# Router logits taken from the product that turns attention outputs back, in a chained attention, expert and feed-forward kernel

## The reference, cut to what matters

```python
y = attention(q, k, v, a_re, a_im)          # 4 batches, 8 heads, 768 positions, 48 columns
x = y.transpose(0, 2, 1, 3).reshape(3072, 384)
do_compute = (x @ w_skip) > 0               # rows that go to an expert
logits = x @ w_gate                         # 8 experts
e_idx = argmax(logits, axis=1)
gate = softmax(logits)[e_idx]
x[do_compute] += gate * (relu(x @ w1[e_idx]) @ w2[e_idx])
h = x @ w_in
out = (h * sigmoid(h)) @ w_out              # 384 -> 2048 -> 384
```

## Time and profile before

| | |
|---|---|
| median of 3 runs | 878.77 us (878.76 to 878.89) |
| the profiled execution | 878.05 us, of which 876.3 us in the span |
| TensorE busy, whole span | 830.9 us (95%) |
| VectorE, ScalarE, GpSimd busy | 357.0, 347.1, 160.6 us |
| mean granted TensorE clock | 0.985 of full speed |
| attention and routing, about | 0 to 298 us |
| experts' first product | from 306.65 us |

### The profile page before, as it was taken

One profiled execution on the slowest core, in us unless ns is written; L12 is line 12 of the kernel. 1 busy time (PEld: TensorE's weight loads), 2 busy tenths in 40 slices (PEclk: granted clock), 3 DMA queues, 4 the chain that ended last, 5 costly groups with the idle time before them and its releaser, 6 DMA issues.

```text
span 876.3 us, 13204 instructions
## 1 busy us (share of the span) xinstructions
PE 830.9 (95%) x5194; PEld 744.6 (85%) x5194; DVE 357.0 (41%) x668; ACT 347.1 (40%) x606; POOL 160.6 (18%) x193
## 2 busy tenths in 40 slices
PE   1499999999999799999999999999999999999997
PEld 0277887798899589999998989998999889988997
DVE  1598878868765422223413122132122122122112
ACT  6889988888652131111112222222222222222221
POOL 2101122712503305555300001001001001001001
PEclk9699999999999899999999999999999999999999
DMA  9999778666523496899720001000000000000001
GB/s 171 160 205 244 105 99 123 113 94 83 136 94 117 140 202 167 266 233 252 224 73 1 1 0 37 1 1 37 1 1 36 1 1 37 1 1 37 0 1 37
DMA packets 174165, 77.31 MB, mean 88 GB/s; under 512 B 151592, under 2 KB 167304, under 8 KB 174096
## 3 DMA queue, kind: packets, MB, share of 16 engines
q1 hardware_dynamic: 169168, 60.54, 34.4%
q0 software_dynamic: 4928, 15.84, 6.4%
HBM read 60.80 MB, written 15.59 MB: 87 GB/s over the span
## 4 chain that ended last, share of the span: by engine, by line
PE 91%; DVE 3%; issue 2%; ACT 2%; DMA 1%; POOL 0%; SPq 0%; DVEq 0%; ACTq 0%; POOLq 0%
PE f_pU L1698 23%; PE f_pO L1704 22%; PE e_pH L1434 9%; PE e_pY L1448 8%; PE sc L515 5%; PE kvp L529 3%; PE tq L497 2%; PE tk L502 2%; PE yp L540 2%; PE yp L542 2%; PE cs L472 2%; PE cs L110 2%; PE cs L485 1%; PE cs L486 1%; PE cs L92 1%
## 5 line engine op out<-in xcount | busy, mean ns | idle before, releaser
L1698 PE MATMUL f_pU<-f_xT,wi 128*128 128x512 f32 x864 | 215.1, 395 | 0.8 <-DVE f_xT L1639 0.8
L1704 PE MATMUL f_pO<-wo,gT 128*128 128x384 f32 x1152 | 213.8, 336 | 0.0
L1704 PEld LDWEIGHTS f_pO<-wo,gT 128*128 128x128 f32 x1152 | 202.6, 188 | 7.5
L1698 PEld LDWEIGHTS f_pU<-f_xT,wi 128*128 128x128 f32 x864 | 161.3, 188 | 32.5 <-DVE f_xT L1639 1.2
L1655 DVE TENSOR_TENSOR gT<-g,gT 128x512 fp32r<-128x512 f32 x96 | 66.5, 692 | 286.5 <-ACT gT L1682 286.5
L1677 ACT ACTIVATE g<-f_pU 128x512 f32<-128x512 f32 x96 | 57.5, 599 | 298.3 <-PE f_pU L1698 298.3
L1645 POOL DMA_INDIRECT out<-o,row_of x24 | 24.1, 1004 | 420.8 <-DVE o L1666 414.4
L1434 PE MATMUL e_pH<-e_xT,ring 128*128 128x224 f32 x384 | 75.8, 358 | 0.1
L1434 PEld LDWEIGHTS e_pH<-e_xT,ring 128*128 128x128 f32 x384 | 74.0, 194 | 0.7 <-issue 0.3
L1448 PE MATMUL e_pY<-hT,ring 128*128 128x224 f32 x384 | 74.1, 353 | 0.0
L1448 PEld LDWEIGHTS e_pY<-hT,ring 128*128 128x128 f32 x384 | 72.1, 190 | 0.0
(11 more groups left out here) (196 smaller groups left out, 1007.6 us busy)
## 6 DMA issues: line engine op xcount, KB each, us to landing
ring<-in_moe_w SPq DMA_DIRECT2D x16, 1536.0 KB, 9.6
ring<-in_a_re SPq DMA_DIRECT2D x8, 576.0 KB, 8.8
ring<-in_a_im SPq DMA_DIRECT2D x8, 576.0 KB, 8.9
ring<-in_q SPq DMA_DIRECT2D x8, 576.0 KB, 8.1
ring<-in_k SPq DMA_DIRECT2D x8, 576.0 KB, 8.2
vraw<-in_v SPq DMA_DIRECT2D x8, 576.0 KB, 5.4
xs<-zero SPq DMA_DIRECT2D x9, 343.9 KB, 7.1
part<-in_moe_w_in POOLq DMA_DIRECT2D x12, 256.0 KB, 6.3
```

The costliest lines, as they stand in the source:

```text
L1698: mm = pe.matmul(pU[f % 2][:, :], wi[:, pw, c, f * 128:(f + 1) * 128], xT[b % 2][:, px, c, :], start=(k == 1), stop=(k == NK * len(TERMS)))
L1704: mm = pe.matmul(pO[t][:, 0:DM], gT[f % GB][:, pg, t * 128:(t + 1) * 128], wo[:, pw, f, :], start=(f == 0 and k == 0), stop=(f == NF - 1 a ...
```

## The change

The turning back of a pair becomes a product with a matrix `back_w` of 105 columns: 96 columns of the identity and behind them 9 columns of the router's weights for this pair's rows of x (`NE` = 9, `TW` = 105). One product then gives the turned-back outputs and the pair's part of the nine numbers. VectorE copies the parts away (`lg_out`), and sums the four parts of a tile in front of `choose`. The tiles' own transposes, copies and logit products go. All 48 steps now turn their outputs back, those of the last period too. `back_w` is filled by GpSimd and by four small loads more.

```diff
     def load(self, sp, s, w_skip, w_gate):
         E = self.E
-        sp.wait_ge(s["wg_blank"], 1)
+        sp.wait_ge(s["wg_blank"], 2)
...
+    def load_pairs(self, sp, s, w_skip, w_gate, back_w, at, half, d):
+
+        for m in range(2):
+            rows = back_w[m * half:m * half + d]
+            sp.dma_start(rows[:, :, at:at + self.E], w_gate.rearrange("(q m d) e -> m d q e", m=2, d=d)[m])\
+                .then_inc(s["wg_in"], 16)
+            sp.dma_start(rows[:, :, at + self.E:at + self.E + 1],
+                         w_skip.rearrange("(q m d o) -> m d q o", m=2, d=d, o=1)[m],
+                         allow_slow_non_contiguous=True).then_inc(s["wg_in"], 16)
...
             load_qk(0)
             load_v(0)
+            routing.load_pairs(sp, s, w_skip, w_gate, back_w, D2, HALF, D)
             load_a(2)
...
+            pool.memset(back_w[:, :, :], 0.0).then_inc(s["wg_blank"], 1)
             routing.constants(pool, s)
+            pool.wait_ge(s["wg_blank"], 1)
+            for m in range(2):
+                eye = back_w[:, :, m * D:(m + 1) * D]
+                pool.affine_select(out=eye, in_=eye, compare_op=ALU.not_equal, fill=1.0, base=-m * HALF,
+                                   pattern=[[0, 2 * PAIRS], [-1, D]], channel_multiplier=1).then_inc(s["const_ok"], 1)
...
+            def tile_here(n):
+                pool.wait_ge(s["x_out"], tile_step(n) + 1)
+
+            def tile_paced(n):
+
+                pool.wait_ge(s["x_out"], max(tile_step(n) + 1, (G - 1) * NC + 1 + n % NC // 2))
...
                 if n >= 3:
-                    pe.wait_ge(s["x_out"], min(n - 2, SWAPPED))
+                    pe.wait_ge(s["lg_out"], n - 2)
...
             def turn_back(n):
-                if not 0 <= n < SWAPPED:
-                    return
-                pe.wait_ge(s["y_out"], n + 1)
-                pe.wait_ge(s["s_out"], n + 2)
-                for i in range(PAIRS):
-                    mm = pe.transpose(back[n % 2][:, i * DP:(i + 1) * DP], YT[n % 2][0:DP, i, :], ident[0:DP, 0:DP])
...
+                g = n // NC
+                pe.wait_ge(s["y_out"], n + 1)
+                pe.wait_ge(s["s_out"], min(n + 2, LAST))
+                if n == 0:
+                    pe.wait_ge(s["wg_in"], 96)
+                    pe.wait_ge(s["const_ok"], 5)
+                if n == LAST - 1:
+                    pe.wait_ge(s["lg_out"], n - 1)
+                for i in range(PAIRS):
+                    mm = pe.matmul(back[n % 2][:, i * TW:(i + 1) * TW], YT[n % 2][0:DP, i, :],
+                                   back_w[0:DP, g % 2 * PAIRS + i, :], start=True, stop=True)
+                mm.then_inc(s["back_turned"], 1)
...
-            logits(X.shape[1] - 2)
-            turn_x(X.shape[1] - 1)
+            turn_back(LAST - 1)
             routing.ranks(pe, s, 4, banks[4])
-            logits(X.shape[1] - 1)
             keep_busy(2)
...
+            def lg_out(n):
+
+                if n < 0:
+                    return
+                if n < LAST - 1:
+                    dve.wait_ge(s["x_out"], n + 1)
+                else:
+                    dve.wait_ge(s["back_turned"], n + 1)
+                dve.tensor_copy(parts(n), back[n % 2][:, 0:PAIRS * TW].rearrange("p (i e) -> p i e", i=PAIRS)[:, :, D2:TW])\
+                    .then_inc(s["lg_out"], 1)
+
+            def choose(b):
+                t, u = routing.batches[b]
+                k = t % NC
+                dve.wait_ge(s["lg_out"], tile_step(t + u - 1) + 1)
+                dve.tensor_reduce(lgs[:, 0:u, :], part_lg[:, t // NC % 2, k:k + u].rearrange("p n q e -> p n e q"), AX.X,
+                                  ALU.add).then_inc(s["lg_sum"], 1)
+                dve.wait_ge(s["lg_sum"], b + 1)
+                routing.choose(dve, s, b, lgs[:, 0:u, :], link)
...
                 for c in range(NC):
                     n = p * NC + c
+                    lg_out(n - 2)
                     state(n)
                     first(p, c)
                     s_out(n + 1)
                     between(p, c)
                     k_out(n + 2)
                     last(p, c)
-            routing.place(dve, s, 4, banks[4], link)
-            routing.choose(dve, s, 5, banks[5], link)
+            lg_out(LAST - 2)
+            lg_out(LAST - 1)
+            choose(5)
             routing.mark(dve, s, 5, link)
             routing.run(dve, s, 5)
+            routing.place(dve, s, 4, banks[4], link)
             routing.place(dve, s, 5, banks[5], link)
```

More of the change, by code:

```diff
@@ L112, in logits, with choose @@
         mm.then_inc(s["logit_done"], 1)
-    def choose(self, dve, s, b, pL, link):
+    def choose(self, dve, s, b, lg, link):
         ALU, AX = mybir.AluOpType, mybir.AxisListType
@@ L173, in place, with scatter @@
         dve.tensor_copy(self.slots[:, t:t + u], self.row[:, t:t + u]).then_inc(s["slot_done"], 1)
-    def scatter(self, pool, s, b, xs, pace=None):
+    def scatter(self, pool, s, b, xs, tile_here=None):
         t, u = self.batches[b]
@@ L179, in scatter @@
         for n in range(t, t + u):
-            if pace is not None and n > t and (n - t) % 2 == 0:
-                pool.wait_ge(s["y_out"], pace + (n - t) // 2)
+            if tile_here is not None:
+                tile_here(n)
             pool.indirect_dma_start(xs, bass.IndirectOffsetOnAxis(ap=self.slots[:, n:n + 1], axis=0), self.X[:, n, :], None,
@@ L337, in attention, with parts, tile_step @@
         back = [sp_[(n + 1) % 2][:, :, :].rearrange("p h c -> p (h c)") for n in range(2)]
+        def parts(n):
+            g, c = n // NC, n % NC
+            return part_lg[:, g // 2 % 2, c, g % 2 * PAIRS:(g % 2 + 1) * PAIRS, :]
+        def tile_step(n):
+            return (n // NC * 2 + 1) * NC + n % NC
         def flat(t):
@@ L446, in gpsimd @@
                 if p in (3, 5, 7):
-                    routing.scatter(pool, s, p // 2 - 1, xs, pace=p * NC + 2 if p == G - 1 else None)
+                    routing.scatter(pool, s, p // 2 - 1, xs, tile_paced if p == G - 1 else tile_here)
                 if p in (2, 4, 6):
@@ L531, in update, with outputs @@
                 mm.then_inc(s["kv_done"], 1)
-            def outputs_turned(n):
+            def outputs(n):
+                if n < 0:
+                    return
                 g, c = n // NC, n % NC
+                if n > 0:
+                    pe.wait_ge(s["y_out"], n)
+                if c > 0:
+                    pe.wait_ge(s["u_done"], g * (NC - 1) + c)
+                pe.wait_ge(s["s_out"], n + 1)
                 for i in range(PAIRS):
@@ L612, in sums @@
                     if c == NC - 1 and j == 2:
+                        pe.wait_ge(s["slot_done"], 3)
                         routing.ranks(pe, s, 3, banks[3])
[L614 to L617, removed]
             def keep_busy(n):
                 for _ in range(n):
-                    pe.matmul(sp_[0][:, 0:NK, :].rearrange("p h c -> p (h c)"), routing.ones,
-                              routing.wg.rearrange("p c e -> p (c e)"), start=True, stop=True)
+                    pe.matmul(yp[:, 0:DM], routing.ones, routing.wg.rearrange("p c e -> p (c e)"), start=True, stop=True)
             pe.matmul(yp[0:SUB, 0:PAIRS * C], zero[:, 0:SUB], zero[:, 0:PAIRS * C], start=True, stop=True)
@@ L809, in scalar @@
                     x_out(n - 1)
-                    if p in (2, 4, 6) and 1 <= c < 4:
-                        xT_out((p // 2 - 1) * NC + 2 * c - 1)
-                    if p == G - 1 and c > 0:
-                        xT_out((G // 2 - 1) * NC + c - 1)
                     after(p, c)
             y_out(LAST - 1)
-            xT_out(X.shape[1] - 1)
+            x_out(LAST - 1)
         def vector(dve):
@@ L1173, in vector @@
             for b in range(NB):
-                routing.choose(dve, s, b, banks[b], link)
+                t, u = routing.batches[b]
+                dve.wait_ge(s["logit_done"], t + u)
+                routing.choose(dve, s, b, banks[b][:, 0:u * (routing.E + 1)].rearrange("p (n e) -> p n e", n=u), link)
                 routing.mark(dve, s, b, link)
```

83 lines of the change are left out of this document (21 added, 62 removed).

## The result

| | before | after |
|---|---|---|
| median | 878.83 us (878.76 to 879.26, 4 runs) | 887.38 us (885.89 to 890.25, 4 runs) |
| ratio | | 1.0100 (95% interval 1.0073 to 1.0127) |
| profiled execution, span | 878.05, 876.3 us | 890.25, 888.5 us |
| mean granted clock | 0.985 | 0.976 |

The kernel became 8.5 us slower; the forecast was 878.6 us, within 874.0 to 882.5. In the span, which falls in the slowest of the four executions, the difference is 12.2 us. I set the terms of the prediction's sum against it. All starts are read as in the earlier trace rows, from the score products (L549 now), p:c being period and step.

What follows compares the result with a forecast made beforehand. TensorE's own work was taken to set the pace, with VectorE having 3.2 us to spare in the shorter period. Terms +2.5, +2.1, 0, -3.6 and -1.2 gave -0.2 us, added to the 878.77 median: 878.6 us, range 874.0 to 882.5.

Steps and rivals of the forecast that it cites:

- TensorE's sum: TensorE's work alone: 24.0 us removed, 4.5 returned, 13.1 added, a gain of 15.4 us; 13 us followed through steps and tail.
- The wait that moves: Score products wait for VectorE's copy of 18 logit columns (0.16 us), first in its next step, behind VectorE's whole step.
- gated step: Step whose score products wait for VectorE's logit copy; 37 of them, 4.24 us each where two half products run.
- the reduce costs 0.15 more: VectorE's sum over four parts ahead of `choose`: 216 elements, put at 0.36 us, plus 0.04 for its wait.
- the step behind `mark`: Step 5 to step 0 of the next period after `mark`: VectorE's 0.80 us more is not hidden, 6.89 us.
- periods 1 to 5: Linear attention's periods 1 to 5, from step 5 to step 5: 155.1 us against 153.0 before, +2.1 us.
- The resumption: VectorE's copy end to score products: 0.10 us; a rival had 0.20, +3.7 us in all, 882.3 us, chance 0.23.
- TensorE idle 1 to 2 us a period at an unchanged clock.: Sign expected in the trace after: TensorE pauses 1 to 2 us each period while its granted clock stays unchanged.
- period 0: First period, from its step 2: score products held up by VectorE, +1.34 and +1.12 us, together +2.5 us.
- the tail: Last period's step 4 to the last scatter's end: 15.7 us before, work removed from its chain, -1.2 us.
- period 7: Last period, steps 0 to 4: 20.03 us before, VectorE has little there, TensorE needs 16.4, -3.6 us.
- What comes behind the last scatter: From the last scatter's end through the experts' part to the kernel's end: no change, 0 us.

Runs made afterwards that it cites:

- products alone: Kernel before, outputs turned back by float32 products with 105 columns of an identity, without router weights, old router kept: 888.12 us, ratio 1.0100.
- copy out of the way: Kernel after, with ScalarE copying the 18 logit columns right behind its own copy of the outputs: 863.15 us, ratio 0.9818.
- Filling the pauses: Kernel after, with ten products that nobody reads put on TensorE where it paused: 884.62 us, ratio 1.0061.
- 16 memsets: Kernel after, with 16 one-column memsets at the head of VectorE's program: 882.62 us, ratio 1.0041.
- the copy in its step: Kernel after, with VectorE's copy of the logit columns taken one step earlier, behind the first half product: 869.95 us, ratio 0.9900.
- padded kernel before: Kernel before, with 54 one-column memsets at the head of VectorE's program: 882.58 us, ratio 1.0040.
- Both repairs at once: Kernel after, with unread products where TensorE paused and 16 one-column memsets at the head of VectorE's program: 881.52 us, ratio 1.0030.
- the wait alone: Kernel before, with VectorE copying 18 unread columns at the head of its next step and the scores waiting for that: 898.64 us, ratio 1.0219.

## Why the prediction was wrong

Its mechanism was right, and its sum held where it was about work and order. Two things that it costed at nothing made the miss.

1. *TensorE's sum.* Right. The products alone cost 9.2 us (10.5 predicted for them in periods 0 to 6), and with the copy out of the way the whole change gains 15.8 us (15.4 by that sum).
2. *The wait that moves.* Right in kind: it eats all the gain. Its size was low. Each gated step has 4.30 us instead of 4.24, the reduce costs 0.15 more, the step behind `mark` 7.03 instead of 6.89: periods 1 to 5 came out at +3.97, not +2.1. The resumption, 0.10 in the forecast and 0.20 in a rival, is 0.14 in the rows.
3. *"TensorE idle 1 to 2 us a period at an unchanged clock."* **This step failed.** In periods 1 to 5 the clock held at 1.00, with 1.6 and 0.6 us of idle time in two of them. In period 0, around S(7:0) and in the tail it did not, and the sum has no term for that. Filling the pauses is worth 2.8 us in the median; in the kernel with 16 memsets it was worth only 1.1 (882.62 to 881.52). In the traces it is 3.4 us: period 0 took +3.30 instead of +4.25 (forecast +2.5), period 7 -3.61 instead of -1.97 (forecast -3.6), the tail -1.34 instead of -0.52 (forecast -1.2). The +1.28 us ahead of S(0:0) is the clock too, in another way: it is larger the later the clock rises behind 41 us. With a mean clock of 0.95 and 0.93 from 45 to 48 us it is +0.43 (pauses filled) and +0.48 (16 memsets), with 0.67 it is +1.28 (after), with 0.62 it is +1.52 (products alone). The edits of the first two touch nothing of TensorE's there, so some 0.8 us of the 1.28 is more likely the chance of the profiled execution than the change; why the clock rises when it does stays open.
4. *What comes behind the last scatter was costed at 0.* **The larger failure**, 4.8 of the 8.5 us by the 16 memsets alone (3.9 by the 54 in the kernel before, 3.1 where the pauses were filled already). The change puts 54 more instructions in front of the experts' part of VectorE's program, which lies behind a jump: it starts behind 1098 instead of 1044 (instructions of the program, those jumped over included; the profile records 453 and 399 operations up to the first reduce). The kernels with 1098 (after, the copy in its step, the filled pauses, the padded kernel before) all show the gap, at the first reduce; the one with 1086 has its first reduce on time and its second, seven recorded operations on, 1.3 us behind its operand, "<-issue" again; those with 1114 and 1144 have none there, nor have those with 1044 and 1050. Sixteen memsets take it away, 54 bring it into the kernel before. The moment doesn't decide: the reduce's operand is ready between 291 and 312 us in the kernels with the gap, and between 290 and 315 in those without. So the place in the program is shown as the cause. That the piece of program behind the seam is fetched late is argued, not shown: in the kernel after the queues for instructions move two packets between 314 and 316 us, amid loads that have filled all 16 engines since 310. With the 16 memsets such packets move too, between 305 and 308 and between 312 and 314 us, and the reduce at 310.49 is on time. DMA queues of 314 to 316 us in the kernel after (packets, MB, share of the engines):

```profile
q1 hardware_dynamic: 320, 0.48, 101.5%
q8 instruction: 1, 0.02, 3.8%
q14 instruction: 1, 0.01, 1.5%
```

   The Trainium skill, page "Runtime: NRT & Kernel Launch", section "Instruction fetch mechanics", states that a program comes in blocks of 256 instructions and that a taken branch breaks the fetching ahead. The late start behind a jump agrees with it; no run here moves the seam by a whole block, so the 256 is not seen. The section calls the cost of crossing from block to block "mostly hidden". If the seam is such a crossing, the gap of 5.2 us in the kernel after does not agree with that.

The account in medians: -0.2 predicted, +1.9 for periods 1 to 5, +2.8 clock, +4.8 seam is +9.3, against +8.5 measured. Both repairs at once took 5.9 us off and not 7.6, so either one of the last two is put too high by its single experiment, or the late copies of the last kernel hid part of the gain.

What would have been possible from the trace of before: the tail of the kernel and each jump could have been asked what lies behind them once instructions are added. Nothing in that trace shows where the seam is, so this would have been a rival with a price, not a term.

## What to carry to other kernels

When a copy that releases a bank changes engine, its place in the new engine's order counts more than its length: the 0.17 us of work at the head of VectorE's next step cost 17.4 us against the same copy in VectorE's own step (887.4 against 870.0, both with the gap at the reduce), and 24 us against the copy on ScalarE (863.2, without the gap). A forecast with pauses of TensorE in it needs a rival in which the work behind them runs at half clock. And before a change of this size is judged by its time, shift an engine's program by a few harmless instructions: here 3 to 5 us hung on that alone.

## What the hardware showed beyond that

- The length of a pause did not tell whether the granted clock would fall to 0.50. In the kernel after it fell behind a wait of 1.24 us, behind one of 1.41 and in the tail behind 0.48, 0.38 and 0.48 us; behind one of 1.84 us that ended at 266.55 it stayed at 1.00 up to 272. In the kernel with 16 memsets nearly the same wait (1.85 us, ended at 266.04) was followed by 0.50 from 268 to 270. With the wait alone, waits of 1.51 and 1.64 us were followed by 0.50 from 285 to 291 us. In periods 1 to 5 of the kernel after no wait (up to 1.00 us) was followed by a fall.
- VectorE stood still for 4.5 to 6.5 us behind a jump with its operands ready (4.5 in the padded kernel before, 4.9 with the pauses filled, 5.2 after, 6.5 with the copy in its step), with 1098 instructions ahead, and not with 1114.
- The reduce of 216 elements, read with a stride, took 0.52 us, where the slope from the earlier trace rows had led me to 0.36.
